# Up and down projections as two 64-row matmul streams, with the down part three steps behind

## The chip, the cores and the metric

The kernel runs on one core of a Trainium2 chip. Its engines work beside each other: TensorE (PE) multiplies, VectorE (DVE), ScalarE (ACT) and GpSimd (POOL) work on elements, SyncE (SP) issues the transfers. The metric is the device time of one execution in microseconds, the median of several. Matrix products take operands from SBUF and write to PSUM, here in banks of 512 float32 columns.

## The reference

```python
w = exp(weight_gen - max) / (sum + 1e-9)              # softmax over 7 taps, per token and head
x_unf = x_pad[:, idx, :].reshape(B, S, 7, 8, 24)      # the token and the 6 before it
x = einsum('bshk,bskhg->bshg', w, x_unf)              # 8192 tokens x 192 features
h = x @ moe_w_in; x = maximum(0.01 * h, h) @ moe_w_out            # 192 -> 2048 -> 192
h = x @ moe2_w_in; out = where(h > 0, h, exp(min(h, 0)) - 1) @ moe2_w_out
```

Batch 2, sequence 4096, width 192, hidden width 2048, all float32.

## The kernel before

Tokens go in 16 chunks (CH) of 512 (T). A phase is one MLP on one chunk: 32 phases of 8 steps (ST); a step handles 256 hidden features as two halves of 128 (`HALF`). `run` sets the order: MLP 1 of chunk c alternates with MLP 2 of chunk c-1; a device loop covers 13 pairs of phases, c from 2 to 14. `g` counts steps through the kernel, `m` is the MLP, `dm` that of the phase before.

Each float32 factor is kept as a rounded part (`_hi`, type fp32r) and a remainder (`_lo`), and a product is the sum of hi*hi, lo*hi and hi*lo. The 192 features are 128 (`in_a`) and 64; `in_b` holds the rounded part of the 64 in its low 64 rows and their remainder in the high ones, `up_b_hi` and `up_b_lo` hold the same 64 weight rows twice. So `up` (L517) is 5 matmuls of 512 columns a half, 10 a step; among them `up_b_lo` times `in_b` includes remainder times remainder. The down part (`down_b` L546, L547, `down_a` L551 to L553) is 5 a half as well: `y_a` takes output features 0 to 127, `y_b` has features 128 to 191 in its low rows and their correction in the high ones.

PE runs `up(g)` and then `down` of step g-2. `hidden` has two buffers in PSUM, `act`, `hid_hi` and `hid_lo` two in SBUF. For each step ACT makes the scaled or exponential part in `act` (L781, or L784 and L786), DVE the nonlinearity, written over `hidden` (L914 or L917), ACT the rounded part `hid_hi` from `hidden` (L811), DVE the remainder `hid_lo` (L953). PE's `up(g)` waits for `s_lo` of g-2.

In step 1 of a phase `take_y` (ACT, L725 and L734) and `add_y` (DVE, L894) empty `y_b` and `y_a` of the phase before; PE waits for them before the first `down` of its phase, in step 2. In MLP 1 phases DVE computes the softmax of the next chunk (`softmax_a` in step 0, `softmax_b` in step 2, L854 to L860). When it is there POOL mixes the seven taps of that chunk (`mixing`, products L284 and adds L296). In step 2 of the MLP 2 phase DVE turns the mix in squares (`turn_mix`, L899), two rounds of transfers through memory put it features first, and `mlp1_input_hi` and `_lo` (steps 5 and 6) make the operands of the next MLP 1 phase. `mlp2_input_hi` and `_lo` (steps 3 and 4, L878 and L880) do this for MLP 2, `turn_back` (L909) turns the output. All engines take their instructions in order. In the first phase the weights of each MLP are split into hi and lo (`round_up`, `round_down` on ACT, `split_up`, `split_down`: L833, L345), and the mix of chunk 1 is transposed on PE after step 6 (`transpose_mix`, L599, L601). `turn_mix` of chunk c stands behind a wait:

```python
dve.wait_ge(s_mix, c + 1)
nc.vector.transpose(prod_sq..., mix...).then_inc(s_mixsq, 1)
```

## Time and profile before

| | us |
|---|---|
| median of 3 runs | 1203.03 (1201.78 to 1203.28) |
| the profiled execution | 1203.83, its span 1202.1 |
| PE, weight loads (PEld) busy | 1183.2, 971.9 |
| DVE, ACT, POOL busy | 783.2, 748.5, 387.5 |
| granted clock of PE, mean | 0.997 |

A line of the page names the line of the kernel, the engine, the operation, output and inputs, how many, their busy time, the mean duration of one and the idle time in front of them with what ended it. Matmuls are pipelined, so a recorded duration is longer than the distance to the next start.

### The profile page before, as it was taken

The numbers are of one execution on the slowest core, as the hardware profiler recorded it, in microseconds if no ns is written. First come the engines' busy times: TensorE is split into PE (matmuls) and PEld (weight loads), VectorE is DVE, ScalarE is ACT, GpSimd is POOL, SyncE is SP. The second block draws the span as 40 slices with busy tenths as digits, with TensorE's granted clock in tenths as the row PEclk, the third lists the DMA queues.
The fourth block names the chain that finished last, engine by engine and source line by source line (L and its number), as shares of the span: only waits on it lengthen the run. The fifth ranks groups of instructions, "written<-read, shape, count | busy, mean of one in ns | idle before, by whom it ended". The sixth has DMA issues, their size and how long they took to land.

```text
span 1202.1 us, 14835 instructions
## 1 busy us (share of the span) xinstructions
PE 1183.2 (98%) x5208; PEld 971.9 (81%) x5208; DVE 783.2 (65%) x778; ACT 748.5 (62%) x815; POOL 387.5 (32%) x411
## 2 busy tenths in 40 slices
PE   7899999999999999999999999999999999999998
PEld 5687888888888888888888888888888888888886
DVE  6877666756667576665766667566665766666555
ACT  3466757566575765657566575665657666575675
POOL 5835080430705216070340805317061250800000
PEclk8999999999999999999999999999999999999999
DMA  6221012021111201012011110201112010100000
GB/s 195 89 73 37 27 41 64 26 64 37 50 26 39 63 26 50 26 39 63 26 57 32 38 51 26 76 26 50 26 39 63 26 50 26 39 26 27 14 26 28
DMA packets 44642, 54.24 MB, mean 45 GB/s; under 512 B 4116, under 2 KB 32914, under 8 KB 44624
## 3 DMA queue, kind: packets, MB, share of 16 engines
q1 hardware_dynamic: 44624, 54.01, 14.5%
q8 instruction: 11, 0.18, 0.1%
q14 instruction: 7, 0.06, 0.0%
HBM read 36.29 MB, written 17.69 MB: 45 GB/s over the span
## 4 chain that ended last, share of the span: by engine, by line
PE 92%; DVE 3%; POOL 3%; ACT 1%; DMA 1%; issue 0%; SPq 0%; POOLq 0%; ACTq 0%
PE hidden L517 45%; PE y_b L546 9%; PE y_a L552 9%; PE y_a L553 9%; PE y_a L551 9%; PE y_b L547 9%; POOL mix L296 1%; DVE hid_lo L953 1%; POOL prod L284 1%; DVE hidden L914 1%; ACT hid_hi L811 1%; DMA xw<-in_x_dram 1%; PE turn L586 0%; PE turn L590 0%; DVE up_b_lo L833 0%
## 5 line engine op out<-in xcount | busy, mean ns | idle before, releaser
L953 DVE TENSOR_TENSOR hid_lo<-hidden,hid_hi 128x1024 fp32r<-128x1024 f32 x254 | 310.8, 1223 | 241.5 <-ACT hid_hi L811 241.5
L811 ACT ACTIVATE hid_hi<-hidden 128x1024 fp32r<-128x1024 f32 x254 | 260.6, 1026 | 270.8 <-DVE hidden L914 143.1
L284 POOL TENSOR_TENSOR mix<-xw,wk 128x384 f32<-128x384 f32 x30 | 26.1, 870 | 640.4 <-DVE wk L860 637.3
L917 DVE SCALAR_TENSOR_TENSOR hidden<-act,hidden 128x1024 f32<-128x1024 f32 x129 | 157.4, 1220 | 104.5 <-ACT act L786 102.4
L517 PE MATMUL hidden<-in_a_hi,up_a_hi 128*128 128x512 f32 x510 | 200.3, 393 | 4.9 <-DVE hid_lo L953 4.3
L546 PE MATMUL y_b<-hid_hi,dn 128*128 128x512 f32 x512 | 199.3, 389 | 0.1
L552 PE MATMUL y_a<-hid_hi,dn 128*128 128x512 f32 x512 | 199.2, 389 | 0.0
L553 PE MATMUL y_a<-hid_lo,dn 128*128 128x512 f32 x512 | 199.2, 389 | 0.0
L547 PE MATMUL y_b<-hid_lo,dn 128*128 128x512 f32 x512 | 199.2, 389 | 0.0
L551 PE MATMUL y_a<-hid_hi,dn 128*128 128x512 f32 x512 | 199.2, 389 | 0.0
L517 PE MATMUL hidden<-in_a_hi,up_a_lo 128*128 128x512 f32 x510 | 198.6, 389 | 0.0
L517 PE MATMUL hidden<-in_b,up_b_hi 128*128 128x512 f32 x510 | 198.6, 389 | 0.0
L517 PE MATMUL hidden<-in_b,up_b_lo 128*128 128x512 f32 x510 | 198.6, 389 | 0.0
L517 PE MATMUL hidden<-in_a_lo,up_a_hi 128*128 128x512 f32 x510 | 198.5, 389 | 0.0
L781 ACT ACTIVATE act<-hidden 128x1024 f32<-128x1024 f32 x127 | 130.6, 1028 | 101.9 <-PE hidden L517 101.7
L296 POOL TENSOR_TENSOR mix<-mix,prod 128x384 f32<-128x384 f32 x180 | 186.8, 1038 | 2.4
L914 DVE TENSOR_TENSOR hidden<-hidden,act 128x1024 f32<-128x1024 f32 (+1 forms) x129 | 157.6, 1222 | 42.2 <-ACT act L781 39.6
L284 POOL TENSOR_TENSOR prod<-xw,wk 128x384 f32<-128x384 f32 x180 | 167.4, 938 | 9.4
L784 ACT ACTIVATE act<-hidden 128x1024 f32<-128x1024 f32 x127 | 130.6, 1029 | 26.1 <-PE hidden L517 17.7
L786 ACT ACTIVATE act<-act 128x1024 f32<-128x1024 f32 x127 | 134.7, 1060 | 4.0
L517 PEld LDWEIGHTS hidden<-in_a_hi,up_a_hi 128*128 128x128 f32 x510 | 95.7, 188 | 30.5 <-issue 7.0
L546 PEld LDWEIGHTS y_b<-hid_hi,dn 128*128 128x128 f32 x512 | 96.1, 188 | 20.5 <-issue 0.5
(100 smaller groups left out, 1103.0 us busy)
## 6 DMA issues: line engine op xcount, KB each, us to landing
xw<-in_x_dram SPq DMA_DIRECT2D x14, 960.0 KB
raw_b<-squares_out SPq DMA_DIRECT2D x60, 96.0 KB, 2.2
out_dram<-staged SPq DMA_DIRECT2D x15, 384.0 KB, 2.4
squares_in<-prod SPq DMA_DIRECT2D x56, 96.0 KB, 2.0
squares_out<-ya SPq DMA_DIRECT2D x15, 256.0 KB, 2.0
raw_a<-squares_in SPq DMA_DIRECT2D x14, 256.0 KB, 2.7
raw_d<-in_moe_w_out_dram SPq DMA_DIRECT2D x8, 384.0 KB, 6.8
raw_a<-in_moe_w_in_dram SPq DMA_DIRECT2D x8, 256.0 KB, 4.1
```

Of the source, the lines that this page charges most:

```text
L284: ops.tensor_tensor(dst, src, w, ALU.mult).then_inc(done, 1)
L296: ops.tensor_tensor(mix[:, j0:j1, :], mix[:, j0:j1, :], terms[k % n][:, j0:j1, :], ALU.add).then_inc(done, 1)
L517: last = nc.tensor.matmul(dst, w[m][:, cols], v[src][:, :], start=(n == 0), stop=(n == len(pairs) - 1))
L546: nc.tensor.matmul(y_b[:, :], dn[m][:, f, P:2 * P], hi, start=(f == 0), stop=False)
L547: return nc.tensor.matmul(y_b[:, :], dn[m][:, f, P:2 * P], lo, start=False, stop=(f == FT - 1))
L551: nc.tensor.matmul(y_a[:, :], dn[m][:, f, 0:P], hi, start=(f == 0), stop=False)
L552: nc.tensor.matmul(y_a[:, :], dn[m][:, f, 2 * P:3 * P], hi, start=False, stop=False)
L553: return nc.tensor.matmul(y_a[:, :], dn[m][:, f, 0:P], lo, start=False, stop=(f == FT - 1))
L811: nc.scalar.activation(hid_hi[:, s % 2, :], hidden[:, s % 2, :], ACT.Copy).then_inc(s_hi, 1)
L914: nc.vector.tensor_tensor(h, h, a, ALU.max).then_inc(done, 1)
L917: nc.vector.scalar_tensor_tensor(out=h, in0=a, scalar=-1.0, in1=h, op0=ALU.add, op1=ALU.max).then_inc(done, 1)
L953: nc.vector.tensor_tensor(hid_lo[:, s % 2, :], h, hid_hi[:, s % 2, :].bitcast(f32), ALU.subtract).then_inc(s_lo, 1)
```

## The change

- Every matmul of the loop takes 64 of the 128 rows, low or high; the two streams alternate in PE's program and write different PSUM banks at any time. `up` has 18 matmuls: 12 for the three products with `in_a`, 4 for `up_b_hi`, 2 for `up_b_lo`. `up_b_lo` is multiplied with the rounded part alone, for which `in_b_up` holds it in the high rows also (an extra 64-row copy on ACT for each input).
- The down part has 20 matmuls. `y_a` gets two banks, one for each half of the rows, and one more add on DVE. `turn` shrinks to one bank.
- The down part is that of step g-3. It is cut in two: first half of up, `down_open`, second half of up, `down_close`; in step 2 the order is up, open, close, up. `hid_hi` and `hid_lo` get four buffers.
- The nonlinearity goes into `act`; rounding and remainder read `act`, so `hidden` is free (`s_g`) once the nonlinearity is done. Rounding of step g-1 stands behind the activation of step g.
- `take_y` and `add_y` go to step 2, `turn_mix` to step 1, the operands of MLP 1 to steps 4 and 5, `turn_back` to step 6. PE waits for the emptied banks in step 3.
- The raw weight buffers are half as large, and each load waits for a split.

```diff
+    LAG = 3
+    HB = 4
...
-        up_b_lo = [sb(f"up_b_lo{m}", [P, F], f32r) for m in (0, 1)]
+        up_b_lo = [sb(f"up_b_lo{m}", [P, F // 2], f32r) for m in (0, 1)]
...
-        raw_d = sb("raw_d", [P, FT, D], f32)
+        raw_d = sb("raw_d", [P, FT // 2, D], f32)
...
+        in_b_up = [sb(f"in_b_up{n}", [P, T], f32r) for n in (0, 1)]
...
-        hid_hi = sb("hid_hi", [P, 2, 2 * T], f32r)
-        hid_lo = sb("hid_lo", [P, 2, 2 * T], f32r)
+        hid_hi = sb("hid_hi", [P, HB, 2 * T], f32r)
+        hid_lo = sb("hid_lo", [P, HB, 2 * T], f32r)
...
-        y_a = ps("y_a", [P, T])
+        y_a = [ps(f"y_a_rows{h}", [P, T]) for h in (0, 1)]
         y_b = ps("y_b", [P, T])
-        turn = ps("turn", [P, 2, T])
-        turn_cols = turn[:, :, :].rearrange("p a (q j t) -> p a j q t", q=Q, j=J)
+        turn = ps("turn", [P, T])
+        out_turn = hidden[:, 0, :]
...
-            load_weights(0, moe_w_in, moe_w_out)
+            load_up(0, 0)
+            load_up(0, 1)
+            load_down(0, 0)
+            load_down(0, 1)
...
-            load_weights(1, moe2_w_in, moe2_w_out)
+            load_up(0, 2)
+            load_up(0, 3)
+            load_down(0, 2)
+            load_up(1, 0)
+            load_up(1, 1)
+            load_down(0, 3)
+            load_down(1, 0)
+            load_down(1, 1)
+            load_up(1, 2)
...
-            def up(m, src, g, s):
-                for i in (0, 1):
+            LOW, HIGH = slice(0, D2), slice(D2, P)
+
+            def up(m, src, g, s, second):
+
+                def up_a(rows, i, n, stop=False):
+                    w, v = ((up_a_hi, in_a_hi), (up_a_lo, in_a_hi), (up_a_hi, in_a_lo))[n]
                     cols = slice((2 * s + i) * P, (2 * s + i + 1) * P)
-                    dst = hidden[:, s % 2, i * T:(i + 1) * T]
-                    pairs = ((up_a_hi, in_a_hi), (up_a_lo, in_a_hi), (up_b_hi, in_b), (up_b_lo, in_b), (up_a_hi, in_a_lo))
-                    for n, (w, v) in enumerate(pairs):
-                        last = nc.tensor.matmul(dst, w[m][:, cols], v[src][:, :], start=(n == 0), stop=(n == len(pairs) - 1))
-                    if halved(g) and i == 0:
-                        last.then_inc(s_up1, 1)
-                last.then_inc(s_up, 1)
+                    start = n == 0 and i == (0 if rows == LOW else 1)
+                    return nc.tensor.matmul(hidden[:, s % 2, HALF[i]], w[m][rows, cols], v[src][rows, :], start=start, stop=stop)
+
+                def up_b(rows, i, stop=False):
+                    cols = slice((2 * s + i) * P, (2 * s + i + 1) * P)
+                    return nc.tensor.matmul(hidden[:, s % 2, HALF[i]], up_b_hi[m][rows, cols], in_b[src][rows, :], start=False, stop=stop)
+
+                if not second:
+                    for n in range(3):
+                        up_a(LOW, 0, n)
+                        up_a(HIGH, 1, n)
+                    up_b(LOW, 0)
+                    up_b(HIGH, 1)
+                    up_pair(m, src, s)[1].then_inc(s_open, 1)
+                    return
+
+                pe.wait_ge(s_open, g)
+                for n in range(3):
+                    up_a(LOW, 1, n)
+                    up_a(HIGH, 0, n)
+                half1 = up_b(LOW, 1, stop=True)
+                half0 = up_b(HIGH, 0, stop=True)
+                if halved(g):
+                    half0.then_inc(s_up1, 1)
+                    half1.then_inc(s_up, 1)
+                else:
+                    half0.then_inc(s_up, 1)
+
...
+            def up_pair(m, src, s, stop=False):
+                cols = slice(s * P, (s + 1) * P)
+                low = nc.tensor.matmul(hidden[:, s % 2, HALF[0]], up_b_lo[m][LOW, cols], in_b[src][LOW, :], start=False, stop=stop)
+                high = nc.tensor.matmul(hidden[:, s % 2, HALF[1]], up_b_lo[m][HIGH, cols], in_b_up[src][HIGH, :], start=False, stop=stop)
+                return low, high
...
+            def down_b(m, s, rows, i, n):
+
+                f = 2 * s + i
+                v = (hid_hi, hid_lo)[n]
+                start, stop = f == 0 and n == 0 and rows == LOW, f == FT - 1 and n == 1 and rows == HIGH
+                return nc.tensor.matmul(y_b[:, :], dn[m][rows, f, P:2 * P], v[rows, s % HB, HALF[i]], start=start, stop=stop)
...
+            def down_a(m, s, rows, i, n):
+
+                f = 2 * s + i
+                first, v = ((0, hid_hi), (2 * P, hid_hi), (0, hid_lo))[n]
+                bank = y_a[0] if rows == LOW else y_a[1]
+                return nc.tensor.matmul(bank[:, :], dn[m][rows, f, first:first + P], v[rows, s % HB, HALF[i]],
+                                        start=(f == 0 and n == 0), stop=(f == FT - 1 and n == 2))
...
+            def down_open(m, s, d, starts=None):
+
+                if starts is not None:
+
+                    pe.wait_ge(s_yb, starts)
+                    pe.wait_ge(s_ya1, starts)
+                if not (known(d) and d == 0):
+
+                    pe.wait_ge(s_dn, d)
+                down_b(m, s, LOW, 0, 0)
+                down_a(m, s, HIGH, 0, 0)
+                down_b(m, s, LOW, 0, 1)
+                down_a(m, s, HIGH, 0, 1)
+                down_b(m, s, LOW, 1, 0)
+                down_a(m, s, HIGH, 0, 2)
+                down_b(m, s, LOW, 1, 1).then_inc(s_yblow, 1)
+                down_a(m, s, HIGH, 1, 0)
+                if starts is not None:
+
+                    pe.wait_ge(s_ya, starts)
+                down_a(m, s, LOW, 0, 0)
+                down_a(m, s, HIGH, 1, 1)
+
+            def down_close(m, s, d):
+
+                down_a(m, s, LOW, 0, 1)
+                down_a(m, s, HIGH, 1, 2)
+
+                down_a(m, s, LOW, 0, 2)
+                pe.wait_ge(s_yblow, d + 1)
+                down_b(m, s, HIGH, 0, 0)
+                down_a(m, s, LOW, 1, 0)
+                down_b(m, s, HIGH, 0, 1)
+                down_a(m, s, LOW, 1, 1)
+                down_b(m, s, HIGH, 1, 0)
+                down_a(m, s, LOW, 1, 2)
+                down_b(m, s, HIGH, 1, 1).then_inc(s_dn, 1)

             def down_last():

                 s = ST - 1
-                for i in (0, 1):
...
-                        pe.wait_ge(s_lo, g - 1)
-                    up(m, input_of(m, c), g, s)
-                    if known(ph) and ph in (0, 2) and s in (2, 4, 6, 7):
...
+                        pe.wait_ge(s_g, g - 1)
+                    up(m, input_of(m, c), g, s, False)
...
+                    pe.wait_ge(s_lo, g - LAG + 1)
+                    down_open(of, step, g - LAG, ph if s == LAG and dm is not None else None)
+                    if s == LAG - 1:
+
+                        down_close(of, step, g - LAG)
+                        up(m, input_of(m, c), g, s, True)
                     else:
-                        if s == 2 and dm is not None:
-
...
+            for d in range(LAG - 1, 0, -1):
+                pe.wait_ge(s_lo, END - d + 1)
+                down_open(1, ST - 1 - d, END - d)
+                down_close(1, ST - 1 - d, END - d)
...
+                    nc.scalar.activation(in_b_up[input_of(1, c)][D2:P, :], yb[0][:, :], ACT.Copy)
...
+            def rounding(g, s):
+
+                act_e.wait_ge(s_g, g + 1)
+                if not (known(g) and g < HB):
+
+                    act_e.wait_ge(s_dn, g + 1 - HB)
+                nc.scalar.activation(hid_hi[:, s % HB, :], act[:, s % 2, :], ACT.Copy).then_inc(s_hi, 1)
...
+                    if s == LAG - 1 and dm is not None:
                         take_y(dm, dc, ph - 1)
-                    if m == 1 and s in (5, 6) and not (known(c) and c >= CH - 2):
-                        mlp1_input_hi(c + 2, s - 5)
+                    activation(m, c, g, s)
+                    rounding(g - 1, (s - 1) % ST)
+                    if m:
+                        exponential(c, s)
+                    if m == 1 and s in (4, 5) and not (known(c) and c >= CH - 2):
+                        mlp1_input_hi(c + 2, s - 4)
                     if m == 0 and s in (3, 4) and not (known(c) and c == 0):
...
+                dve.wait_ge(s_ya1, ph + 1)
+                a0, a1 = y_a[0][:, :], ya[dm][:, :]
+                if known(ph) and ph == LAST:
+                    a0, a1 = last_columns(a0, False), last_columns(a1, True)
+                nc.vector.tensor_tensor(a1, a0, a1, ALU.add).then_inc(s_ya, 1)
...
+            def rests(g, s):
+
+                dve.wait_ge(s_hi, g + 1)
+                nc.vector.tensor_tensor(hid_lo[:, s % HB, :], act[:, s % 2, :], hid_hi[:, s % HB, :].bitcast(f32), ALU.subtract).then_inc(s_lo, 1)
...
+                    if s == LAG - 1 and dm is not None:
                         add_y(dm, dc, ph - 1)
+                    if m == 0:
+                        activation(m, g, s)
+                        rests(g - 1, (s - 1) % ST)
+                    else:
+                        rests(g - 1, (s - 1) % ST)
+                        activation(m, g, s)
...
-                    if m == 1 and s == 2 and not (known(c) and c >= CH - 2):
+                    if m == 1 and s == 1 and not (known(c) and c >= CH - 2):
                         turn_mix(c + 2)
-                    if m == 1 and s in (5, 6) and not (known(c) and c >= CH - 2):
-                        mlp1_input_lo(c + 2, s - 5)
-                    if s == 5 and dm == 1:
+                    if m == 1 and s in (4, 5) and not (known(c) and c >= CH - 2):
+                        mlp1_input_lo(c + 2, s - 4)
+                    if s == 6 and dm == 1:
                         turn_back(dc)
```

## Rows read from the trace of the kernel before

**Rows 1.** The page: busy time by engine, and the chain that ended last by engine.

```profile
PE 1183.2 (98%) x5208; PEld 971.9 (81%) x5208; DVE 783.2 (65%) x778; ACT 748.5 (62%) x815; POOL 387.5 (32%) x411
...
PE 92%; DVE 3%; POOL 3%; ACT 1%; DMA 1%; issue 0%; SPq 0%; POOLq 0%; ACTq 0%
```

**Rows 2.** Waits of PE: line waited for, us in total, times, longest.

```profile
PE hidden L517 <- DVE hid_lo L953: 4.3, 7, 1.3
...
PE turn L599 <- POOLq L490: 1.8, 1, 1.8
```

**Rows 3.** Windows, one loop turn: length, busy PE, PEld, DVE, ACT, POOL, clock, DMA.

```profile
284.00:356.60 72.60, 72.60 (x321) 59.97 (x321) 46.94 (x46) 45.73 (x50) 24.46 (x26) 1.00 0.14 42
```

**Rows 4.** Timeline, steady down part: start, us, engine line op, forms.

```profile
600.24 0.39 PE L552 MATMUL y_a<-hid_hi,dn 128*128 128x512 f32 x1
600.24 0.19 PEld L553 LDWEIGHTS y_a<-hid_lo,dn 128*128 128x128 f32 x1
600.46 0.39 PE L553 MATMUL y_a<-hid_lo,dn 128*128 128x512 f32 x1
```

**Rows 5.** Timeline, weight loads of the first mix from 17.66 us, four merged.

```profile
17.65 0.52 PEld L586 LDWEIGHTS turn<-ident,mix 128*128 128x128 f32 x4 [0.17 <-issue]
```

**Rows 6.** Timeline, last transposes: a 128-row matmul and a 64-row one.

```profile
1197.23 0.33 PE L610 MATMUL turn<-ident,ya 128*128 128x128 f32 x1 [0.75 <-ACT ya L734]
...
1197.49 0.27 PE L611 MATMUL turn<-ident,yb 64*128 64x64 f32 x1
```

**Rows 7.** Timeline, first weight load of a loop turn.

```profile
283.95 0.19 PEld L517 LDWEIGHTS hidden<-in_a_hi,up_a_hi 128*128 128x128 f32 x1 [0.23 <-issue]
```

**Rows 8.** Lines by form: count, busy us, mean ns, idle before.

```profile
L953 DVE TENSOR_TENSOR hid_lo<-hidden,hid_hi 128x1024 fp32r<-128x1024 f32 x254 | 310.8, 1223 | 241.5 <-ACT hid_hi L811 241.5
L811 ACT ACTIVATE hid_hi<-hidden 128x1024 fp32r<-128x1024 f32 x254 | 260.6, 1026 | 270.8 <-DVE hidden L914 143.1 <-DVE hidden L917 127.6
...
L786 ACT ACTIVATE act<-act 128x1024 f32<-128x1024 f32 x127 | 134.7, 1060 | 4.0
```

**Rows 9.** Timeline, two SBUF inputs on DVE: POOL silent, then POOL mixing.

```profile
22.10 0.68 DVE L833 TENSOR_TENSOR up_a_lo<-raw_a,up_a_hi 128x512 fp32r<-128x512 f32 x1
...
304.16 1.01 POOL L296 TENSOR_TENSOR mix<-mix,prod 128x384 f32<-128x384 f32 x1
304.68 1.04 DVE L878 TENSOR_TENSOR in_a_lo<-ya,in_a_hi 128x512 fp32r<-128x512 f32 x1
305.25 1.20 POOL L284 TENSOR_TENSOR prod<-xw,wk 128x384 f32<-128x384 f32 x1
...
309.43 1.32 POOL L284 TENSOR_TENSOR prod<-xw,wk 128x384 f32<-128x384 f32 x1
```

**Rows 10.** Timeline, first softmax_b piece; first and last POOL instructions of a chunk.

```profile
298.15 0.38 DVE L854 TENSOR_REDUCE wsum<-wk 128x32 f32<-128x224 f32 x1
...
299.79 0.87 POOL L284 TENSOR_TENSOR mix<-xw,wk 128x384 f32<-128x384 f32 x1 [47.37 <-DVE wk L860]
...
322.93 2.10 POOL L296 TENSOR_TENSOR mix<-mix,prod 128x384 f32<-128x384 f32 x2
```

**Rows 11.** Timeline, copy and add of y_b, and the transpose of the mix.

```profile
293.43 0.59 ACT L725 ACTIVATE ylow<-y_b 64x512 f32<-64x512 f32 x1 [1.32 <-PE y_a L553]
...
294.15 0.68 DVE L894 TENSOR_TENSOR yb<-y_b,ylow 64x512 f32<-64x512 f32 x1 [0.77 <-ACT ylow L725]
...
337.50 0.97 DVE L899 STREAM_TRANSPOSE prod<-mix 128x768 f32<-128x768 f32 x1
```

**Rows 12.** Timeline of the start, and a weight load's us to landing (page).

```profile
58.19 0.66 PE L599 MATMUL turn<-ident,mix 128*128 128x128 f32 x4 [1.81 <-POOLq L490]
...
59.04 0.48 PE L517 MATMUL hidden<-in_a_hi,up_a_hi 128*128 128x512 f32 x1
...
raw_a<-in_moe_w_in_dram SPq DMA_DIRECT2D x8, 256.0 KB, 4.1
```

**Rows 13.** Timeline of the end, the last copy.

```profile
1196.58 0.60 ACT L734 ACTIVATE ya<-y_a 128x512 f32<-128x512 f32 x1 [0.82 <-PE y_a L553]
```

More of the change, by code:

```diff
@@ L549, in down_a @@
-            def down_a(m, f, hi, lo):
-                nc.tensor.matmul(y_a[:, :], dn[m][:, f, 0:P], hi, start=(f == 0), stop=False)
-                nc.tensor.matmul(y_a[:, :], dn[m][:, f, 2 * P:3 * P], hi, start=False, stop=False)
-                return nc.tensor.matmul(y_a[:, :], dn[m][:, f, 0:P], lo, start=False, stop=(f == FT - 1))
-            def down(m, s):
-                for i in (0, 1):
-                    hi, lo = hid_hi[:, s % 2, HALF[i]], hid_lo[:, s % 2, HALF[i]]
-                    down_b(m, 2 * s + i, hi, lo)
-                    last = down_a(m, 2 * s + i, hi, lo)
-                last.then_inc(s_dn, 1)
+                low, high = up_pair(0, input_of(0, 0), 0, stop=True)
@@ L574, in sum_first_mix @@
             def sum_first_mix():
                 pe.wait_ge(s_zero, 1)
-                for bank, rows in ((0, P), (1, D2)):
-                    nc.tensor.matmul(turn[0:rows, bank, :], zeros[:, 0:rows], zeros[:, :], start=True, stop=False)
+                turn_a, turn_b = transposed(0)
+                nc.tensor.matmul(turn_a, zeros[:, 0:P], zeros[:, :], start=True, stop=False)
+                nc.tensor.matmul(turn_b, zeros[:, 0:D2], zeros[:, :], start=True, stop=False)
                 for term, steps in FIRST_TERMS:
@@ L585, in sum_first_mix @@
                     for j in range(J):
-                        last = nc.tensor.matmul(turn_cols[:, 0, j], term[:, j, 0:P], ident[:, :], start=False, stop=(end and j == J - 1))
+                        last = nc.tensor.matmul(by_token(turn_a)[:, j], term[:, j, 0:P], ident[:, :], start=False, stop=(end and j == J - 1))
                     if end:
@@ L589, in sum_first_mix, with transpose_mix @@
                     for j in range(J):
-                        last = nc.tensor.matmul(turn_cols[0:D2, 1, j], term[:, j, P:D], ident[:, :], start=False, stop=(end and j == J - 1))
+                        last = nc.tensor.matmul(by_token(turn_b)[:, j], term[:, j, P:D], ident[:, :], start=False, stop=(end and j == J - 1))
                     last.then_inc(s_mixt if end else s_termu, 1)
-            def transpose_mix(c):
+            def transpose_mix(c, part):
                 pe.wait_ge(s_mix, c + 1)
-                pe.wait_ge(s_xin, 2 * c)
+                pe.wait_ge(s_xin, 2 * c + part)
+                first, last_col = (0, P) if part == 0 else (P, D)
                 for j in range(J):
-                    nc.tensor.transpose(turn_cols[:, 0, j], mix[:, j, 0:P], ident[:, :])
-                for j in range(J):
-                    last = nc.tensor.transpose(turn_cols[0:D2, 1, j], mix[:, j, P:D], ident[:, :])
+                    last = nc.tensor.transpose(by_token(transposed(c)[part])[:, j], mix[:, j, first:last_col], ident[:, :])
                 last.then_inc(s_mixt, 1)
@@ new lines, in activation, with exponential @@
+            def activation(m, c, g, s):
+                act_e.wait_ge(s_up, g + 1)
+                if not (known(g) and g < 2):
+                    act_e.wait_ge(s_lo, g - 1)
+                if m == 0:
+                    nc.scalar.activation(act[:, s % 2, :], hidden[:, s % 2, :], ACT.Copy, scale=SLOPE).then_inc(s_act, 1)
+                else:
+                    nc.scalar.activation(act[:, s % 2, :], hidden[:, s % 2, :], ACT.Relu, scale=-1.0).then_inc(s_relu, 1)
+            def exponential(c, s):
+                act_e.wait_ge(s_relu, ST * c + s + 1)
+                nc.scalar.activation(act[:, s % 2, :], act[:, s % 2, :], ACT.Exp, scale=-1.0).then_inc(s_act, 1)
@@ L805, in phase @@
                             round_down(1, DN2_AT.index((ph, s)))
-                    act_e.wait_ge(s_g, g + 1)
-                    if not (known(ph) and ph == 0 and s < 2):
-                        act_e.wait_ge(s_dn, g - 1)
-                    nc.scalar.activation(hid_hi[:, s % 2, :], hidden[:, s % 2, :], ACT.Copy).then_inc(s_hi, 1)
             softmax_exp(0)
```

327 lines of the change are left out of this document (186 added, 141 removed).

## The prediction

> **What bounds the kernel now.** I began with the page: TensorE (PE) is busy 98% of the span and the chain that ended last is 92% PE, nearly all of it matmuls of 512 columns [rows 1]. Next the waits of PE: in steady work it waits for nobody, 4.3 us in all for the remainder of the hidden block, and 1.8 us once for GpSimd (POOL) in the start [rows 2]. Then one turn of the loop, from 284.0 to 356.6 us, two phases of 8 steps: 72.60 us, all of it PE [rows 3]. Sixteen steps of 20 matmuls are 320 matmuls, so one costs 226.7 ns from start to start (the recorded 0.39 us overlaps with the next, and its 0.19 us weight load begins with the matmul before it [rows 4]). I call 226.7 ns a slot; a step is 20 slots, 4.53 us. VectorE (DVE) and ScalarE (ACT) use 46.9 and 45.7 us of that turn, POOL 24.5 [rows 3]. PE's slot count sets the time; only what makes PE wait can add to it.
>
> **Slots.** The up part of a step goes from 10 full matmuls to 18 half ones, which are 9 slots if a low-row and a high-row matmul run side by side; the product of two low-order parts is gone. The down part goes from 10 to 20 half ones, 10 slots. So 19 slots a step, 4.307 us at 226.7 ns. No row shows two 64-row streams at once, so the slot must be bounded. Below: 512 columns at full clock (the 2.4 GHz level, granted through the steady part [rows 3]) are 213 ns, so 13 ns of a slot are something else; if the second stream hides them, a slot is about 216. Above: each slot now holds two weight loads of 128 columns. Four of them followed each other in 0.52 us with 0.19 for the last, 0.11 us apart [rows 5]; two are 0.22 us, just inside a slot. If instead the 13 ns are paid by each matmul, a slot is 240 ns, and 19 x 240 = 4.56 us is a little more than today. I take 226.7, as weight loads at 110 ns still fit and the full matmul pays its 13 ns once per row. The Trainium skill (TensorE: Matmul & The Clock Gate, Part 3) says that matmuls of different row groups start about 4 ns apart and run at once, which by itself gives the same 19 slots. A 64-row matmul after a 128-row one started late, 0.26 us after a 128-column one [rows 6], but all matmuls of the loop have 64 rows.
> From the second phase on 248 steps each lose a slot: 248 x 0.2267 = -56.2 us. The 0.23 us gap at each turn of the loop, where PE waited for a late wait value beside DVE's last input piece [rows 7], should shrink, as that piece comes a step earlier: 11 x 0.08 = -0.9.
>
> **Work off PE, and the port.** Rounding moves from PSUM to the act buffer in SBUF: 1.03 us [rows 8] becomes like the exponential that already reads SBUF there, 1.06 [rows 8]; the additional 64-row copies are 0.6 us a phase on ACT, the additional y_a add 0.7 on DVE. What matters is DVE's remainder. Today `hid_lo <- hidden, hid_hi` has one input in PSUM and takes 1223 ns whatever POOL does [rows 8]. After the change both inputs are in SBUF. Rows 9 show what such an instruction meets while POOL mixes: `in_a_lo <- ya, in_a_hi`, 512 elements, takes 1.04 us instead of the 0.68 of the same shape with POOL silent [rows 9], because it began in the middle of a POOL add that ended at 305.17; and POOL's next product takes 1.20 and, after the second input piece, 1.32, instead of the 0.87 of [rows 10]. So each stands still while the other works: DVE waits for the rest of a POOL instruction (0 to 0.8 us, mean about 0.45), and POOL loses 0.33 and 0.45, mean 0.40, for a DVE instruction of 0.68. The remainder is 0.54 us longer, so POOL loses 0.94 us for each. The Trainium skill (SBUF - State Buffer, Who interferes with whom) states it as a rule: the shared pair is locked for a whole instruction, and a DVE instruction with two SBUF inputs takes it against a GpSimd one that reads SBUF; by that rule the trace agrees.
>
> **The new wait.** POOL mixes chunk c+1 from 299.79 to 325.03 (last two adds from 322.93, 2.10) [rows 10], 25.24 us, started by the last softmax piece that began with the reduce at 298.15. DVE takes the result with the transpose at 337.50 [rows 11]: 12.5 us of room. After the change:
> - Start. In step 2 of the first phase the order on PE is up, down, down, up, and the down part's end comes at slot 15 of the third step: 2 x 4.307 + 3.29 + 0.39 = 12.29 us after the phase began. ACT then makes two copies (0.59 each, as the one in [rows 11]), act(2) by 14.6, DVE's max to 15.85, remainder to 17.0, softmax from 16.9. POOL starts 1.64 later [rows 10], at 18.54 (today 299.79 - 283.95 = 15.8).
> - Length. Seven remainders (steps 2 to 8) fall in it: 25.24 + 7 x 0.94 = 31.8; POOL ends at 50.4.
> - The transpose stands one step earlier, behind the nonlinearity of step 1 of the second phase. Step 9's up part ends at slot 14, 9.737 x 4.307 = 41.9 us; relu, rounding, exponential, and DVE's two instructions bring DVE to it at 47.3 (today 53.5).
> So DVE stands at the transpose for 3.1 us. Behind it in DVE's order are the two adds that empty y_b and y_a, the remainder of step 9 and the nonlinearity of step 10. POOL's end + 0.2 + transpose 0.97 + first add 0.68 [rows 11] + 0.1 for the hand-overs lets PE's down part of step 11 begin at 52.3. PE is there at 11 x 4.307 + 5 slots = 48.5. Stall: 3.84 us, once in each of the 14 pairs of phases with such a transpose: +53.8 us. With POOL's loss at 0.65 each it is 1.8 us, at 1.22 (the whole instruction) 5.8. A turn of the loop is then 68.9 + 3.8 = 72.7 us beside 72.6: the slot gained in every step is given back in one place.
> - The other two such phases stall without POOL, as two copies, two adds and three ACT passes come in a row: 0.5 us each, +1.0.
>
> **Start and end.** In the start PE waits for POOL's mixing of chunk 1 before the transposes at 58.19 [rows 12]. That mixing begins 1.1 us earlier (a rounding shorter before the softmax) but meets five remainders, +4.7: up(7) begins at 62.6 instead of 59.04. Behind it are one more down part (2.27) and one more group of transposes (0.55), less the shorter step (0.2): +6.2 us. Weights come through half-size buffers, each load behind a split; I cost that at nothing because POOL is later still; uncovered it is one load, 4.1 us to landing [rows 12]. At the end the last copy (0.60 at 1196.58 [rows 13]) is followed by DVE's add of 0.68 before the transposes, +0.75, and each of the last three down parts waits for the one before to leave the array, 0.39 less the slot [rows 4] and a hand-over, 0.25: together +1.5.
>
> **Sum**, against the profiled execution's 1203.8 us (span 1202.1, 0.8 above the median 1203.0): -56.2 - 0.9 + 53.8 + 1.0 + 6.2 + 1.5 = +5.4, 1209.2; against the median 1208.4.
>
> **Rivals.**
> - *PE stays the bound.* If the transpose finds the mixing done (fewer remainders meet POOL, or POOL loses under 0.5 us each) only the 0.5 stalls are left: 1203.0 - 57.1 + 16 x 0.5 + 7.7 = 1162. For it: POOL idles 47.4 us of each turn [rows 10]. Against: the transpose moves 6.2 us towards it and POOL starts 2.7 later. It decides below a loss of 0.5 us. 0.20.
> - *Shorter slot*, 216 ns: the POOL chain fixes all but 8.9 steps of a turn, so 14 x 8.9 x 0.2 = 25 us less, 1184. 0.08.
> - *Slot of 240 ns*, each half matmul paying its own 13: a step 4.56; the turn is POOL's chain plus 8.9 x 0.25, so 14 x 2.3 more than forecast, 1240. From 238.6 the change can't gain at all. 0.13.
> - *Weight loads of the two halves exposed*: the second begins 0.11 after the first and lasts 0.19 [rows 5, 4], slot 298: 256 x (19 x 0.298 - 4.53) = +290, near 1493. 0.08. The Trainium skill (the same page, Measured speedup vs the span model) has four row tiles at 3.07 times one, 77%, and by that a slot is an estimated 295 ns; no row here bears it out.
> - *No overlap at all*: 38 slots a step, 256 x 18 x 0.2267 = +1045, near 2250. 0.06.
> - *Forecast*: 0.45, own range 1185 to 1232 (POOL's loss 0.7 to 1.1).
>
> **Numbers.** A measurement of this kernel can tell about 0.2%, 2.4 us. Faster by more: 0.18 of the forecast's 0.45, the first two rivals 0.28, together 0.46. Within: 0.06. Slower: 0.21 + 0.27 = 0.48. The range 1150 to 1262 leaves out the exposed loads, no overlap and a little of the first rivals, 0.17.
>
> **What would show it.** In the profile after: matmuls of one row half 227 ns apart with those of the other half between them; the remainder at 1.22 to 2.0 us while POOL works; POOL's busy time up by some 90 us; DVE waiting 3 us before each transpose of `mix` for POOL; PE waiting once a turn before the down part of step 3 for `yb`. A half-stream cadence far from 227, or a transpose that doesn't wait, makes the prediction wrong.

## The result and the profile after

| | before | after |
|---|---|---|
| median of the runs | 1202.8 us (1201.8 to 1203.3) | 1236.0 us (1235.7 to 1236.4) |
| ratio to before, 95% interval | | 1.0277 [1.0259, 1.0295] |
| span of the profiled execution | 1202.1 us | 1234.6 us |
| turn of the loop (two phases) | 72.63 us | 72.8, 74.4 or 75.3 us |

The kernel became 2.8% slower. The forecast was 0.45% slower, 1208.4 us; the range reached to 1262, its part for the forecast's own mechanism to 1232. Three parts of the page of after first. Busy times stand as in [rows 1], and the groups are the costliest ones of one line:

```profile
PE 1156.0 (94%) x9808; PEld 1007.4 (82%) x9808; DVE 828.8 (67%) x817; ACT 740.3 (60%) x846; POOL 486.8 (39%) x411
...
PEclk9999999999999899899999999899899999999999
...
L1116 DVE TENSOR_TENSOR hid_lo<-act,hid_hi 128x1024 fp32r<-128x1024 f32 x255 | 338.5, 1328 | 217.0 <-ACT hid_hi L908 217.0
```

PE's share fell from 98 to 94%: it waits now. The remainder takes 1328 ns where it took 1223 [rows 8], POOL is busy 99 us longer than in [rows 1], and the row of the clock has eights where the kernel before has none in the loop. The waits of after (line waited for, us in total, times, longest) name the new wait and what it hangs on:

```profile
DVE prod L1071 <- POOLq L520: 47.1, 13, 3.6
PE y_b L610 <- issue: 46.5, 13, 3.6
```

One such place, on each engine in turn (start, us, what, idle before and who ended it). First PE, matmuls of one step and the down part that waits; then DVE; then POOL's last instructions of the chunk:

```profile
196.08 0.39 PE L549 MATMUL hidden<-in_a_lo,up_a_hi 64*128 64x512 f32 x2
196.31 0.39 PE L553 MATMUL hidden<-in_b,up_b_hi 64*128 64x512 f32 x2
196.53 0.39 PE L578 MATMUL hidden<-in_b,up_b_lo 64*128 64x512 f32 x1
196.54 0.39 PE L579 MATMUL hidden<-in_b_up,up_b_lo 64*128 64x512 f32 x1
...
200.50 0.46 PE L610 MATMUL y_b<-hid_hi,dn 64*128 64x512 f32 x1 [3.58 <-issue]
```
```profile
198.85 0.98 DVE L1071 STREAM_TRANSPOSE prod<-mix 128x768 f32<-128x768 f32 x1 [3.63 <-POOLq L520]
199.76 0.64 DVE L1060 TENSOR_TENSOR yb<-y_b,ylow 64x512 f32<-64x512 f32 x1
```
```profile
196.70 2.07 POOL L323 TENSOR_TENSOR mix<-mix,prod 128x384 f32<-128x384 f32 x2
```

Two half matmuls now start in one slot, 0.01 us apart, and the slots are 0.226 us from start to start. POOL ends at 198.77, DVE's transpose starts at 198.85 after 3.63 us of standing, the first add ends at 200.40, and PE's down part of step 3 starts at 200.50 after 3.58 us. "Issue" as the releaser of PE hides that last step; the times show it, and in experiment 6, where PE works up to the end of the wait, its trace names the add.

The turns themselves, 13 windows one after the other (window, length, busy PE, clock; the first six shown):

```profile
148.35:221.10 72.75, 69.17 (x612) 1.00 0.14 44
221.10:295.50 74.40, 70.82 (x612) 0.98 0.14 41
295.50:369.85 74.35, 70.77 (x612) 0.98 0.13 41
369.85:445.20 75.35, 71.77 (x612) 0.95 0.13 41
445.20:520.40 75.20, 71.63 (x612) 0.95 0.13 41
520.40:593.20 72.80, 69.22 (x612) 1.00 0.14 42
```

In a turn at clock 1.00 PE is busy 69.17 us and the turn lasts 72.75, nearly the 72.7 forecast. In ten of the 13 turns the clock is below 1.00, PE needs up to 2.6 us more for the same 612 recorded groups, and the turn is that much longer. Where in the turn that happens is seen beside one of the waits (busy PE, PEld, DVE, ACT, POOL, then clock):

```profile
343.00:347.80 4.80, 1.22 (x12) 0.77 (x10) 1.79 (x3) 3.18 (x4) 2.82 (x3) 1.00 0.16 31
347.80:352.40 4.60, 4.60 (x28) 4.26 (x30) 2.62 (x3) 1.61 (x2) 0.00 (x0) 0.63 0.92 285
```
```profile
347.66 0.46 PE L610 MATMUL y_b<-hid_hi,dn 64*128 64x512 f32 x1 [3.58 <-issue]
...
349.64 0.69 PE L549 MATMUL hidden<-in_a_lo,up_a_hi 64*128 64x512 f32 x2
350.06 0.69 PE L553 MATMUL hidden<-in_b,up_b_hi 64*128 64x512 f32 x2
```

The wait ends at 347.66 at full clock; 1.35 us later the clock is at its lower level (1.2 GHz), and pairs start 0.42 us apart instead of 0.23. A mean of 0.63 over 4.60 us between the levels 1.0 and 0.5 is 4.6 x 0.37 x 2 = 3.4 us at the lower one. The six turns of 74.4 us look like this, with the fall 0.6 to 1.4 us after the wait.

In the four turns of 75.2 to 75.4 us the fall comes earlier, while PE still stands. The next turn (busy PE, clock, then the first matmul after the wait):

```profile
415.00:420.70 5.70, 3.50 (x32) 1.00 0.00 0
420.70:427.50 6.80, 5.42 (x26) 0.50 0.75 219
```
```profile
422.08 0.76 PE L610 MATMUL y_b<-hid_hi,dn 64*128 64x512 f32 x1 [3.58 <-issue]
```

The clock is at its lower level from 420.7, 1.4 us before the wait ends, and for 6.8 us in all. PE works in 5.4 of them, and half of that, 2.7 us, is about what the turn is longer.

**Where the 32.5 us of the span came from**, in the order of the forecast:

| | forecast | measured |
|---|---|---|
| start, up to the first up part of phase 1 | +6.2 | +9.8 |
| 13 turns with the new wait, at full clock | +1.9 | 13 x (72.77 - 72.63) = +1.8 |
| lower clock in ten of them | 0 | 965.75 - 13 x 72.77 = +19.7 |
| first and last turn, end | -2.7 | +1.2 |
| sum | +5.4 | +32.5 |

The forecast's sum is split here as it was made: a turn loses 16 slots of 0.2267, 3.63 us, and gains a stall of 3.84, which with the shorter loop gaps is +1.9 for 13 turns; the slots of the other phases, the fourteenth stall, the 0.5 us stalls and the end make -2.7. 965.75 us is the length of the 13 turns together. The start is read from the first up part of phase 1 in the timelines of after (73.50) and before (63.68):

```profile
73.50 0.50 PE L549 MATMUL hidden<-in_a_hi,up_a_hi 64*128 64x512 f32 x2 [1.41 <-DVE in_b L1037]
```
```profile
63.68 0.39 PE L517 MATMUL hidden<-in_a_hi,up_a_hi 128*128 128x512 f32 x1
```

### The profile page after: what moved, and what is told of

Same layout as the page of the kernel before. It is cut to its first block, busy times and chain, and to the rows that moved or that the text cites. A ratio compares the mean times of both kernels' runs of the same rounds, so it can differ in the third digit from the quotient of the medians.

```text
span 1234.6 us, 24425 instructions
## 1 busy us (share of the span) xinstructions
PE 1156.0 (94%) x9808; PEld 1007.4 (82%) x9808; DVE 828.8 (67%) x817; ACT 740.3 (60%) x846; POOL 486.8 (39%) x411
## 4 chain that ended last, share of the span: by engine, by line
PE 86%; issue 5%; DVE 4%; POOL 4%; ACT 1%; DMA 1%; SPq 0%; POOLq 0%
PE y_a_rows L617 27%; PE hidden L549 27%; PE y_b L610 19%; PE hidden L553 9%; PE hidden L578 4%; DVE hid_lo L1116 1%; POOL mix L323 1%; POOL prod L311 1%; PE hidden L579 1%; DVE act L1086 1%; DMA xw<-in_x_dram 1%; DVE up_b_lo L998 0%; DVE act L1089 0%; POOL prod L336 0%; DVE up_a_lo L988 0%
## 5 line engine op out<-in xcount | busy, mean ns | idle before, releaser
L617 PE MATMUL y_a_rows<-hid_hi,dn 64*128 64x512 f32 x2048 | 577.0, 394 | 0.0
L1116 DVE TENSOR_TENSOR hid_lo<-act,hid_hi 128x1024 fp32r<-128x1024 f32 x255 | 338.5, 1328 | 217.0 <-ACT hid_hi L908 217.0
L610 PE MATMUL y_b<-hid_hi,dn 64*128 64x512 f32 x1024 | 403.3, 394 | 50.4 <-issue 46.5
L610 PE MATMUL y_b<-hid_lo,dn 64*128 64x512 f32 x1024 | 400.3, 391 | 0.0
L617 PEld LDWEIGHTS y_a_rows<-hid_hi,dn 64*128 64x128 f32 x2048 | 339.8, 188 | 26.6
L617 PE MATMUL y_a_rows<-hid_lo,dn 64*128 64x512 f32 x1024 | 355.8, 392 | 0.0
L908 ACT ACTIVATE hid_hi<-act 128x1024 fp32r<-128x1024 f32 x255 | 268.3, 1052 | 1.7 <-DVE act L1089 1.5
L311 POOL TENSOR_TENSOR mix<-xw,wk 128x384 f32<-128x384 f32 x30 | 27.1, 904 | 579.9 <-DVE wk L1026 577.0
L549 PE MATMUL hidden<-in_a_hi,up_a_hi 64*128 64x512 f32 x1020 | 211.2, 395 | 10.5 <-DVE act L1086 5.8
L1086 DVE TENSOR_TENSOR act<-hidden,act 128x1024 f32<-128x1024 f32 (+1 forms) x129 | 156.7, 1215 | 89.1 <-ACT act L893 88.9
L323 POOL TENSOR_TENSOR mix<-mix,prod 128x384 f32<-128x384 f32 x180 | 209.2, 1162 | 2.4
L549 PE MATMUL hidden<-in_a_hi,up_a_lo 64*128 64x512 f32 x1020 | 209.8, 392 | 0.0
L549 PE MATMUL hidden<-in_a_lo,up_a_hi 64*128 64x512 f32 x1020 | 209.8, 392 | 0.0
L1089 DVE SCALAR_TENSOR_TENSOR act<-act,hidden 128x1024 f32<-128x1024 f32 x129 | 155.3, 1204 | 0.5 <-ACT act L927 0.5
```

What stands on the lines that cost most here:

```text
L311: ops.tensor_tensor(dst, src, w, ALU.mult).then_inc(done, 1)
L323: ops.tensor_tensor(mix[:, j0:j1, :], mix[:, j0:j1, :], terms[k % n][:, j0:j1, :], ALU.add).then_inc(done, 1)
L549: return nc.tensor.matmul(hidden[:, s % 2, HALF[i]], w[m][rows, cols], v[src][rows, :], start=start, stop=stop)
L610: return nc.tensor.matmul(y_b[:, :], dn[m][rows, f, P:2 * P], v[rows, s % HB, HALF[i]], start=start, stop=stop)
L617: return nc.tensor.matmul(bank[:, :], dn[m][rows, f, first:first + P], v[rows, s % HB, HALF[i]], start=(f == 0 and n == 0), stop=(f == FT ...
L908: nc.scalar.activation(hid_hi[:, s % HB, :], act[:, s % 2, :], ACT.Copy).then_inc(s_hi, 1)
```

## The experiments

Theory A is the forecast's chain with the clock added: remainders with two SBUF inputs hold POOL up, POOL ends late, DVE stands at the transpose, PE stands at the down part of step 3, and after that wait the clock falls. Each run tests one link. All times are beside runs of the kernel before on the same chip, 1202.8 to 1203.1 us.

**1. POOL started a step earlier.**

```diff
-                    if m == 0 and s == 2 and not (known(c) and c in (0, CH - 1)):
+                    if m == 0 and s == 1 and not (known(c) and c in (0, CH - 1)):
                         softmax_b(c + 1)
```

> The changed kernel with softmax_b one step earlier (step 1 instead of 2 of each MLP 1 phase); nothing left out. Theory A (DVE stands at the transpose of the mix because POOL, slowed by the port, ends late; the two adds behind it hold PE; the clock then falls): POOL starts some 5.6 us earlier in each turn, ends before DVE arrives, PE's 3.6 us wait goes and with it the stretches at half clock; a turn falls from 74.4 to about 69.4 us, 14 turns, time 1236 - 14 x 5 = about 1166. Theory B (the banks of y_a and y_b are emptied too late by their own chain of two copies and two adds, whatever POOL does): no change, 1236. Theory C (the clock falls because of the 64-row streams or the transfers, not the wait): the wait goes but the half-clock stretches stay, about 1188.

Measured: 1175.4 us, ratio to before 0.9767 [0.9751, 0.9784]. This one step is worth 61 us: 2.3% faster than before instead of 2.8% slower. DVE's wait at the transpose is gone, the loop runs at full clock and a turn is 69.6 us (the window of one turn, busy PE, clock):

```profile
496.50:566.10 69.60, 69.17 (x610) 1.00 0.13 44
```

What is left beside 16 x 4.307 = 68.9 is mostly a wait of some 0.5 us at the up part of step 4 in MLP 2's phase, where ACT's two copies and three passes come in a row. The start is as long as in after. The expected 1166 was 9 us too low: it took 5 us off 14 turns, but only 13 had the wait, and with it they lasted 74.3 us on average, so that 69.6 takes off 4.7 in each, 61 us.

**2. POOL started a step later.**

```diff
-                    if m == 0 and s == 2 and not (known(c) and c in (0, CH - 1)):
+                    if m == 0 and s == 3 and not (known(c) and c in (0, CH - 1)):
                         softmax_b(c + 1)
```

> The changed kernel with the second softmax part one step later (step 3 of MLP 1's phase instead of step 2). POOL's mixing then starts one step, 8 slots of 0.227 = about 4 us less what the step after differs, later. Theory A (POOL's end sets VectorE's transpose, that sets TensorE's wait): TensorE's wait of 3.6 us a turn grows to about 3.6 + 4.3 = 7.9 us, so a turn without clock falls is 72.8 + 4.3 = 77.1 us and 14 turns add 60 us; with the falls of the clock as before, 1236 + 60 = about 1296 us. Theory C (the wait comes from elsewhere and only coincides with POOL): unchanged, about 1236 us. How much of a turn runs at the half clock after a longer wait I do not know; at least as much as after 3.6 us.

Measured: 1269.8 us, 1.0562 [1.0544, 1.0579]. The direction is theory A's, the size is not: the wait grew by 1.9 us, not 4.3.

```profile
477.85 1.09 POOL L311 TENSOR_TENSOR mix<-xw,wk 128x384 f32<-128x384 f32 x1 [46.71 <-DVE wk L1026]
...
506.38 2.06 POOL L323 TENSOR_TENSOR mix<-mix,prod 128x384 f32<-128x384 f32 x2
```
```profile
DVE prod L1071 <- POOLq L520: 73.3, 14, 5.5
```

POOL starts 22.0 us after its phase began (455.9) instead of 18.4, 3.6 later; and its chunk takes 30.6 us where after needs 32.1, since six remainders fall into it where after has seven: the next ones stand behind DVE's wait. 3.6 - 1.5 leaves 2.1. So the wait damps itself: a POOL that is late meets nothing more once DVE waits for it. The clock is below full in each turn of this kernel, where after had turns without a fall; one of them:

```profile
490.40:566.60 76.20, 70.65 (x610) 0.96 0.13 40
```

**3. Five of POOL's seven taps.**

```diff
+        POOL_TAPS = 5
-        MIX_STEPS = 2 * TAPS - 1
+        MIX_STEPS = 2 * POOL_TAPS - 1
...
-            for k in range(1, TAPS):
-                if k + 1 < TAPS:
+            for k in range(1, POOL_TAPS):
+                if k + 1 < POOL_TAPS:
```

> The changed kernel with POOL's mixing of chunks 1 to 15 cut to 5 of the 7 taps (18 instructions a chunk instead of 26); the last two taps are left out of the sum. Theory A: POOL's 31 us become 22, it ends before DVE arrives, DVE does not wait, PE does not wait, the clock stays full: about 1166, like the earlier softmax, and the start 3 to 7 us shorter too, as PE waits there for POOL: 1160. Theory B: 1236 less the start's few us.

Measured: 1167.6 us, 0.9705 [0.9688, 0.9721]. With less work on POOL, and nothing moved, the wait is gone and the turn is the same 69.6. The start is 6.5 us shorter than in after too:

```profile
67.04 0.49 PE L550 MATMUL hidden<-in_a_hi,up_a_hi 64*128 64x512 f32 x2 [1.41 <-DVE in_b L1038]
```

So POOL's length is on the path in the loop and in the start. The expected 1160 builds on the 1166 of experiment 1 and is too low for the same reason. This run can't say what made it late.

**4. One SBUF input for the remainder.** The loop's remainder subtracts a PSUM bank in place of the rounded value; what `hid_lo` holds there is then wrong, and the run is good for times only.

```diff
-                nc.vector.tensor_tensor(hid_lo[:, s % HB, :], act[:, s % 2, :], hid_hi[:, s % HB, :].bitcast(f32), ALU.subtract).then_inc(s_lo, 1)
+                r, a = hid_hi[:, s % HB, :].bitcast(f32), act[:, s % 2, :]
+                out = hid_lo[:, s % HB, :]
+                if not known(g):
+                    out, a = (x.rearrange("p (i t) -> p i t", i=2) for x in (out, a))
+                    r = turn[:, :].unsqueeze(1).broadcast_to((P, 2, T))
+                nc.vector.tensor_tensor(out, a, r, ALU.subtract).then_inc(s_lo, 1)
```

> The changed kernel, with softmax where the change has it (step 2), but in the loop the remainder subtracts a PSUM bank (broadcast over both halves) in place of the rounded activation in SBUF, so that VectorE reads one operand from SBUF, not two; the low part of the activation is therefore not what the reference needs, in the loop alone. Theory A (two SBUF operands on VectorE keep POOL from the SBUF port): POOL's mixing window of 32.1 us shrinks to about 26 us as before the change, VectorE's 3.6 us at the transpose goes, the turn is 69 to 69.6 us, no fall of the clock; about 1175 us. Rival (the later place of the softmax and the earlier transpose alone cause it, the port does not matter): the wait of 3.6 us stays, 1236 us.

Measured: 1176.3 us, 0.9773 [0.9757, 0.9789]. Order, waits and amount of work are those of after; only the place of one input differs. POOL's groups between 490 and 720 us (busy us, mean ns), first of after, then of this kernel, and this kernel's first and last POOL instruction of a chunk:

```profile
L311 POOL TENSOR_TENSOR prod<-xw,wk 128x384 f32<-128x384 f32 x38 | 52.3, 1382 | 2.0
L323 POOL TENSOR_TENSOR mix<-mix,prod 128x384 f32<-128x384 f32 x39 | 43.8, 1122 | 0.6
```
```profile
L323 POOL TENSOR_TENSOR mix<-mix,prod 128x384 f32<-128x384 f32 x36 | 38.0, 1056 | 0.5
L311 POOL TENSOR_TENSOR prod<-xw,wk 128x384 f32<-128x384 f32 x36 | 31.9, 893 | 1.9
...
447.15 0.87 POOL L311 TENSOR_TENSOR mix<-xw,wk 128x384 f32<-128x384 f32 x1 [44.37 <-DVE wk L1026]
...
470.30 2.11 POOL L323 TENSOR_TENSOR mix<-mix,prod 128x384 f32<-128x384 f32 x2
```

The product falls from 1382 to 893 ns, the chunk from 32.1 to 25.3 us, as long as before the change (25.24). No wait at the transpose is left, no fall of the clock in the loop, 69.6 us a turn. The second SBUF input makes the mixing 6.8 us longer, and without that there is no wait. It is not enough by itself: POOL also starts 2.6 us later than before the change and the transpose stands a step earlier, and where one of these or both are taken back (experiments 1 and 5, and 8) the longer mixing makes no wait at the transpose in the loop either. The Trainium skill (SBUF - State Buffer, Who interferes with whom) says that a DVE instruction with two SBUF inputs contends with a GpSimd one that reads SBUF, and one with at most one such input doesn't: this run shows both halves.

**5. The transpose back in step 2.**

```diff
-                    if m == 1 and s == 1 and not (known(c) and c >= CH - 2):
+                    if m == 1 and s == 2 and not (known(c) and c >= CH - 2):
                         turn_mix(c + 2)
-                    if m == 1 and s in (4, 5) and not (known(c) and c >= CH - 2):
-                        mlp1_input_lo(c + 2, s - 4)
+                    if m == 1 and s in (5, 6) and not (known(c) and c >= CH - 2):
+                        mlp1_input_lo(c + 2, s - 5)
```

(and the same steps for ACT's part of that input.)

> The changed kernel with the transpose of the mixing result back in step 2 of MLP 2's phase and what hangs on it in steps 5 and 6, instead of 1, 4 and 5. Theory A: VectorE reaches the transpose one step, about 4.3 us, later, after POOL has ended (it missed it by 3.6 us), so neither VectorE nor TensorE waits; turn 69.1 to 69.6 us, no fall of the clock, about 1175 us if what hangs on the transpose is still in time for MLP 1 of the next but one chunk. Rival: the input of MLP 1 now comes too late, and TensorE waits at the turn of the phase instead: over 1180 us, with a wait at the first up part of MLP 1.

Measured: 1185.7 us, 0.9860 [0.9844, 0.9877]. No wait for POOL at the transpose, full clock in the loop. But a turn is 70.36 us, 0.7 more than in experiment 1. One of these places, POOL, then DVE, then PE at the up part of step 4:

```profile
550.05 2.11 POOL L323 TENSOR_TENSOR mix<-mix,prod 128x384 f32<-128x384 f32 x2
```
```profile
551.46 1.78 DVE L1116 TENSOR_TENSOR hid_lo<-act,hid_hi 128x1024 fp32r<-128x1024 f32 x1 [1.17 <-ACT hid_hi L908]
```
```profile
554.43 0.50 PE L549 MATMUL hidden<-in_a_hi,up_a_hi 64*128 64x512 f32 x2 [0.99 <-DVE act L1089]
```

PE waits 0.99 us here, where experiment 1 has 0.43 at the same step: there POOL ended before the remainder of that step, here it is still adding, and the remainder takes 1.78 us instead of 1.23. So the time is the rival's (over 1180) and the place is not, and neither theory's price came whole: the input of MLP 1 is in time and POOL is done before the transpose, but DVE meets POOL's last instructions just ahead of a bank that PE needs. The 0.56 us more of this wait are most of the 0.7; what costs the rest I did not trace.

**6. Matmuls during the wait.** The wait stays, but PE isn't idle in it.

```diff
+    FILL = 15
...
                     pe.wait_ge(s_lo, g - LAG + 1)
+                    if m == 1 and s == LAG and not (known(c) and c >= CH - 2):
+                        for _ in range(FILL):
+                            nc.tensor.matmul(turn[:, :], up_a_hi[m][LOW, 0:P], in_a_hi[input_of(m, c)][LOW, :], start=True, stop=True)
                     down_open(of, step, g - LAG, ph if s == LAG and dm is not None else None)
```

> The changed kernel with 15 additional 64-row matmuls into the unused bank of turn, in front of the waits of step 3 of the MLP 2 phases that have a transpose of the mix: 3.4 us of work in place of nearly all of the 3.6 us wait. Nothing that is computed changes. Theory A: DVE's wait of 3.6 us at the transpose stays, the turn stays at 72.8 us where the clock was full, but the half-clock stretches behind the wait go; time about 1236 - 22 = 1214. Theory C (clock falls for another reason): 1236 or a little more. If the fill itself costs time because the wait is shorter than thought: above 1236.

Measured: 1219.2 us, 1.0139 [1.0122, 1.0156]. DVE still stands 3.7 us at each transpose; PE, busy to the end of it, keeps its clock, and its short rest of a wait is now put down to DVE's add of y_b (waits, then one turn):

```profile
DVE prod L1075 <- POOLq L521: 47.5, 13, 3.7
...
PE y_b L611 <- DVE yb L1064: 2.1, 13, 0.2
```
```profile
296.00:368.80 72.80, 72.64 (x627) 1.00 0.14 42
```

All turns are 72.8. The gain on after, 16.8 us, is the 19.7 of the table less 2.4 us that the filler costs in the first turn (77.1 instead of 74.8), where there was no wait for it to fill. This splits the loss: in the loop the wait alone gives back what the slots won, as forecast (72.8 us a turn beside 72.63), and the clock's fall comes on top. The 10.8 us that are left to the forecast's 1208.4 are the filler's 2.4 and, for the most part, the start and the end (below).

**7. The same in the start**, with experiment 1's softmax.

```diff
+            def fill(n):
+                for _ in range(n):
+                    nc.tensor.matmul(turn[:, :], up_a_hi[0][LOW, 0:P], in_a_hi[input_of(0, 0)][LOW, :], start=True, stop=True)
...
+                    if known(ph) and ph == 0 and s in (4, 5):
+                        fill(5)
...
+                    if known(ph) and ph == 0 and s == 5:
+                        fill(10)
...
+                    if known(ph) and ph == 0 and s == 6:
+                        fill(18)
```

> The kernel with softmax in step 1, and beside it filler matmuls into a free bank in the first phase, ahead of the four waits of TensorE there that are over 1.5 us (5 before steps 4 and 5, 10 before the down part of step 5, 18 before the transposes). Half clock in the start was 13.7 us in that kernel; matmuls that ran at it took twice their time, so at most half of it, 6.8 us, is won. Theory (the clock falls after TensorE's waits): the half clock of the start mostly goes and the time falls from 1175.4 to about 1171 us. Rival (VectorE and POOL set the start, TensorE's clock does not matter there): phase 1 begins at 73.9 us as before and the time stays within 1 us of 1175.4.

Measured: 1175.6 us, 0.9776 [0.9760, 0.9792], no gain on experiment 1. PE's clock in the start rose from 0.87 to 0.97 (windows of the first phase, experiment 1 then this one), and the first up part of phase 1 came at 73.45:

```profile
22.60:73.90 51.30, 39.68 (x269) 0.87 0.28 88
```
```profile
22.70:73.50 50.80, 45.29 (x307) 0.97 0.30 89
...
73.45 0.50 PE L549 MATMUL hidden<-in_a_hi,up_a_hi 64*128 64x512 f32 x2 [1.38 <-DVE in_b L1047]
```

The rival stands: in the start other engines set the time, and PE's clock is free there.

**8. Only the SBUF inputs, in the kernel before.** The nonlinearity writes `act`, rounding and remainder read it; all else is the kernel before, but for ACT's first pass, which must now wait for the remainder of two steps before (`act` is read until then); no wait of ACT for it is in the trace.

```diff
-                    nc.vector.tensor_tensor(h, h, a, ALU.max).then_inc(done, 1)
+                    nc.vector.tensor_tensor(a, h, a, ALU.max).then_inc(done, 1)
...
-                    nc.scalar.activation(hid_hi[:, s % 2, :], hidden[:, s % 2, :], ACT.Copy).then_inc(s_hi, 1)
+                    nc.scalar.activation(hid_hi[:, s % 2, :], act[:, s % 2, :], ACT.Copy).then_inc(s_hi, 1)
...
-                    nc.vector.tensor_tensor(hid_lo[:, s % 2, :], h, hid_hi[:, s % 2, :].bitcast(f32), ALU.subtract).then_inc(s_lo, 1)
+                    nc.vector.tensor_tensor(hid_lo[:, s % 2, :], act[:, s % 2, :], hid_hi[:, s % 2, :].bitcast(f32), ALU.subtract).then_inc(s_lo, 1)
```

> The kernel before with one part of the change alone: the nonlinearity goes into act, and rounding and remainder read act (the remainder has two SBUF inputs), everything else as before. Theory A: POOL's busy time goes up from 387 to about 480 us and the remainder's mean from 1223 to about 1330 ns, as each waits for the other, but DVE comes to the transpose 12.5 us after POOL today, so nothing waits there: PE bound, 1203 plus up to 6 in the start, where PE waits for POOL. A rival that says the port costs PE time by itself: 1215 or more.

Measured: 1213.4 us, 1.0085 [1.0068, 1.0102].

```profile
PE 1186.2 (98%) x5208; PEld 972.9 (80%) x5208; DVE 816.9 (67%) x778; ACT 754.3 (62%) x815; POOL 480.3 (40%) x411
...
L953 DVE TENSOR_TENSOR hid_lo<-act,hid_hi 128x1024 fp32r<-128x1024 f32 x254 | 333.6, 1313 | 249.5 <-ACT hid_hi L811 249.5
```

POOL's 93 us more and the remainder's 1313 ns are nearly those of after (99 and 1328), a chunk is mixed in 31.6 us instead of 25.24, and the steady turn doesn't mind: 72.67 us, as its 12.5 us of room take the 6.4 of a longer mixing. The cost is in the start: phase 1 begins 4.5 us later and the first turn is 4.5 longer (79.5 instead of 75.0). So the second input costs 9 us (10.3 by the medians, where up to 6 were expected) even where nothing in the loop waits for POOL. If the changed kernel's start pays the same, about 4.5 of its 9.8 us are from there; no run takes the input away in that start alone.

## Why the prediction was right and wrong

**Slots, right.** 226.7 ns for a pair of half matmuls, 19 to a step: PE is busy 69.17 us of a turn, against 16 x 4.307 = 68.9. The rivals with slots of 216, 240 and 298 ns, and no overlap at all, are out: pairs start 0.226 us apart, and the two weight loads of each are hidden in that. The Trainium skill's four row tiles at 77% (TensorE: Matmul & The Clock Gate, Measured speedup vs the span model) don't carry over to two: the loss here is too small for the timeline to show.

**POOL's lateness, right, and its cause shown.** Forecast for the chunk 31.8 us, measured 32.1; start at 18.54, measured 18.4; wait of DVE 3.1, measured 3.63; wait of PE 3.84, measured 3.58; turn 72.7, measured 72.77; POOL busier by 90, measured 99. Experiment 4 shows that the second SBUF input makes the mixing longer, 1 and 3 that POOL's end decides.

**The clock, the step that failed.** The slots paragraph takes the full clock that is "granted through the steady part" of the kernel before, where PE never waited, and the sum carried that into a kernel for which the next paragraph forecast 3.8 us of idle PE in each turn. The sum has no term for what the clock does after the wait. It was 0; measured, it is 19.7 us, 19.7 of the 27.1 us between forecast and measured span. Experiment 6 shows that it is the idle PE: same wait on DVE, PE kept busy, no fall.

**Start, 3.6 us too small.** I priced the second group of transposes by its 0.55 us on PE. It stands behind step 7's up part, and what it feeds stands in ACT's and DVE's queues behind other work (after, timeline):

```profile
68.97 0.63 PE L716 MATMUL turn<-ident,mix 128*64 128x128 f32 x4
```
```profile
68.87 1.05 ACT L908 ACTIVATE hid_hi<-act 128x1024 fp32r<-128x1024 f32 x1
69.81 0.62 ACT L801 ACTIVATE up_a_hi<-raw_a 128x512 fp32r<-128x512 f32 x1
70.33 0.62 ACT L803 ACTIVATE up_b_hi<-raw_b 128x512 fp32r<-128x512 f32 x1
70.98 0.59 ACT L832 ACTIVATE in_b_up<-turn 64x512 fp32r<-64x512 f32 x1
```

The copies wait for a rounding of an activation and two of weights, DVE's low part comes at 72.76, and PE waits 1.41 us for it at 73.50. The part up to the transposes was nearly right (up(7) at 62.6, measured 63.3). That the half-size weight buffers cost nothing held only so far: PE did wait 2.6 us at 48.47 for a split of down weights, and POOL, later still, covered it.

**First and last turn and end, 3.9 us too small.** I have no run of this part alone; the last turn came as forecast (69.6), and the other two share the miss. The first turn should be 75.0 less 16 slots, less one down part that the forecast has in the start (2.27), with its stall 73.0 us; it took 74.8. That stall, the fourteenth, did not come: POOL ended at 123.22, and DVE, busy with the second MLP's weights, reached the transpose at 125.36. In its place PE waited 4.8 us in four places for DVE's nonlinearity (`act`, L1086 and L1089). So what this turn has nearly right is luck: a wait that was priced stayed away, and a larger one that was not priced came. The end is 1.9 us longer than forecast. There the trace shows PE waiting 2.00 us for the last add before the last transposes, where [rows 6] has 0.75, and the clock at its lower level in them (a transpose of 0.33 in [rows 6] takes 0.43 and, in the next two, 0.47):

```profile
1229.09 0.33 PE L726 MATMUL hidden<-ident,ya 128*128 128x128 f32 x1 [2.00 <-DVE ya L1066]
...
1229.56 0.43 PE L726 MATMUL hidden<-ident,ya 128*128 128x128 f32 x1
```

**The rival that PE stays the bound, 1162,** did not come, but it names what the change could be: with the softmax a step earlier it is 1175.4, the best of the whole kernels run here. The 13 us between are the start (4.0 us longer than forecast), the first turn (4.8, of which 3.7 are waits for DVE's nonlinearity, as above), the end (1.9), and 0.2 in each of 13 turns, where the wait costs a little more than the 0.5 that the rival priced.

## What to carry to other kernels

When a forecast puts an idle stretch of some microseconds on TensorE in every turn of a loop, price the clock after it as a term of its own: here 3.6 us of waiting cost 1.6 to 2.5 us more in ten turns of 13. Moving an operand from PSUM to SBUF is not free if it gives VectorE a second SBUF input while GpSimd works: count these instructions inside GpSimd's window, and see where its result is awaited. If a change that saves TensorE slots loses, look for the one hand-over that it made late before dropping it; here one line moved one step was worth 61 us.

## What the hardware did that I had not expected

- The same wait of 3.58 us had three outcomes. In six turns the granted clock went to its lower level 0.6 to 1.4 us *after* PE had taken up work again and stayed there for 3.4 us; in four it fell 1.4 to 1.7 us *before* the wait ended and stayed low for 6.8 us; in three it did not fall. The order is regular: one turn at full clock, two with 3.4 us, two with 6.8, and then the same again (372 us). What sets it was not tried and stays open.
- What such a stretch costs is about half of the part of it in which PE works: 1.6 us for 3.4, and 2.5 for 6.8, of which PE works in 5.2 to 5.4.
- A late GpSimd mends itself in part: with VectorE standing for it, a chunk took 30.6 us instead of 32.1.
